# Attention chains of a fused attention and expert kernel stood in other steps, one step or more for each link

## The chip, the core and the metric

The kernel runs on one core of a Trainium2 chip. The core has five engines that run at their own pace and meet only at semaphores: PE (TensorE, matrix products, with its weight loads PEld), DVE (VectorE), ACT (ScalarE), POOL (GpSimd) and SP (SyncE, which here only starts transfers). The metric is device time of the whole program in microseconds (us); lower is better.

## What is computed

Three stages follow each other. The change concerns the first and what stands beside it.

```python
scores = scale * np.matmul(q, k.transpose(0, 1, 3, 2))    # q, k, v: 4 x 8 x 576 x 64
mask = (rel >= 0) & (rel < 64)                            # each query sees 64 keys
attn = np.exp(scores - max); attn /= attn.sum(-1) + 1e-9
x = (attn @ v) laid out as 2304 x 512
x = (((x @ w1) * (x @ w2)) @ w3) @ w_out                  # w1, w2: 512 x 1024, w3: 1024 x 1024
...
out[n] = gate[n] * relu(x[n] @ ew1[e]) @ ew2[e]           # e: the best of 8 experts of row n
```

## The kernel before

**Precision.** Each large product is done three times with reduced operands: every matrix is split into a high part (the "h" tiles, written by ACT) and a low part (the "l" tiles, the difference, written by DVE or POOL), and lines 479 to 481 multiply high by high, high by low and low by high.

**Stages.** The program has a fold stage and six chunks. The fold stage multiplies w3 by w_out once (16 half products, index i from 0 to 15 in `w_order`, evicted to Wh and Wl), and beside it splits w1 and w2 in eight pieces (`hi_w12` on ACT, then `lo_w12` on DVE or POOL). Each chunk takes 384 rows of x through eight hidden tiles (`hidden_tile`, steps 0 to 7) and six row tiles (`row_tile`, steps 8 to 13). The eight experts follow after the last chunk.

**Attention beside it.** Attention is computed in blocks, four to a stage, called 0 to 3 here. The fold stage computes the four blocks that chunk 0 needs, and each chunk but the last computes those of the next: six stages with attention in all. One block is a chain over all engines: score (PE, L571) -> masks (DVE: L998 twice, L1003, L1006; these write prob and the negative maxima nmx) -> exps (ACT, L812) -> weigh (DVE, L1024 and L1026: sums and their reciprocals) -> normal (POOL, L1430) -> turn (PE, three transposes into bank 4, L583) -> turn_out (DVE, four L1016 from bank 4 to pT) -> value (PE, L595) -> value_hi (ACT, L817) and value_lo (DVE, L1030), which write the block's columns of xT.

**What sets the order.** Seven small tables by step, `scored`, `laid`, `raised`, `weighed`, `turned`, `valued` and the constant `LAST`, say which block's link is issued in which step on each engine: scored for score, laid for masks, raised for exps, weighed for weigh, turned for turn and turn_out, valued for value with its two evictions. Block 0's score stands at the stage's start, block 3's value in the middle of step 13. In the fold stage step e is the product i = e + 2. Each engine runs its instructions strictly in the order in which they are written, so an engine that waits for one link holds back all that stands behind it. `w12_steps` says after which product each of the eight splits of w1 and w2 is issued, and `w12_pool` which of them have their low part on POOL instead of DVE.

**Waits that matter here.** There is one bank for the transposes: turn of a block waits until turn_out of the block before has read it (`pt_ok`), and for normal of its own block (`p_ok`). The score of a block waits until masks of the one before has read the score banks (`masked`). On DVE, weigh stands ahead of turn_out within a step, and in the fold stage both stand behind the low parts of w3 and w1/w2 and behind the eviction of the product (`own()`). SP issues the loads in one fixed order; a load of q and k waits for a score that frees its buffer (`s_done`), a load of v for a value (`o_done`).

Of the kernel before, what the change touches and what calls it, by code (L numbers as in the profile page):

```python
# [37 lines left out]
def build(nc, B, H, S, qk_pairs, v_pairs, w1, w2, w3T_in, w_out, w_outT, w_gates, ew1, ew2, out):  # L38
# [41 lines left out]
    with ctx:  # L80
# [186 lines left out]


        def scored(e):
            return {2: 1, 5: 2, 8: 3}.get(e)  # L270

        def laid(e):
            return {0: 0, 3: 1, 6: 2, 9: 3}.get(e)

        def raised(e):
            return {1: 0, 4: 1, 7: 2, 9: 3}.get(e)

        def weighed(e):
            return {2: 0, 5: 1, 8: 2, 10: 3}.get(e)

        def turned(e):
            return {4: 0, 7: 1, 10: 2, 11: 3}.get(e)

        def valued(e):
            return {6: 0, 9: 1, 12: 2}.get(e)

        LAST = NP - 1

# [36 lines left out]
        def fold_scored(i):  # L325
            return 0 if i == 2 else scored(i - 2)
# [2 lines left out]
        w3_steps = {1: 3, 5: 4, 7: 5, 9: 6, 11: 7}  # L329


        w12_steps = [3, 6, 8, 9, 10, 12, 13, 14]
        w12_pool = (2, 4, 5)
        pool_count = lambda n: sum(i in w12_pool for i in range(n))
        assert len(w12_steps) == 2 * KD

# [10 lines left out]
        def w_count(it, n):  # L347
            return w_order.index((it, n)) + 1
# [28 lines left out]
        @block.sync  # L377
        def _(sp):
            def load_w3(it):
                if it in w3_prev:  # L380
                    sp.wait_ge(W_done, w_count(w3_prev[it], 1))
                sp.dma_start(w3r[w3_buf[it]][:, :], w3T_in[it]).then_inc(w3_loaded(it)[0], 16)

            def load_w12(i):
                _, _, wr, src, kt = w12[i]
                if i >= KD:
                    sp.wait_ge(wo_lo, KF)
                sp.dma_start(wr[:, kt * FF:(kt + 1) * FF], src[kt * P:(kt + 1) * P, :]).then_inc(w12_in[i], 16)

            def load_woT(i):  # L390
                cols = slice(2 * i * DM, (2 * i + 2) * DM)
                sp.dma_start(woT[:, cols], w_outT[i]).then_inc(woT_in[i], 16)

            def load_wo(n, i):
                c = n * (KF // 2) + i
                sp.dma_start(wo[:, c * DM:(c + 1) * DM], w_out[c]).then_inc(wo_in[c], 16)

            load_w3(0)
            load_wo(0, 0)
            load_wo(0, 1)  # L400
            load_w3(1)
            load_wo(0, 2)
            load_wo(0, 3)
            load_w3(2)
            sp.dma_start(wgg[:, :], w_gates).then_inc(wg_in, 16)
            load_woT(0)
            load_woT(1)
            load_w3(3)
            load_woT(2)
            load_woT(3)  # L410

            def load_qk(G):
                if G >= 2:
                    sp.wait_ge(s_done, 2 * (G - 1))
                sp.dma_start(qk[G % 2][:, :], qk_pairs[G]).then_inc(qk_in[G % 2], 16)

            def load_v(G):
                if G >= 2:
                    sp.wait_ge(o_done, G - 1)
                sp.dma_start(vv[G % 2][:, :], v_pairs[G]).then_inc(v_in[G % 2], 16)  # L420

            load_qk(0)
            for i in range(KF // 2):
                load_wo(1, i)
            load_qk(1)
            load_v(0)
            load_w12(0)
            load_v(1)
            load_qk(2)
            load_w12(1)  # L430
            load_w3(4)
            load_qk(3)
            load_w3(6)
            load_w12(2)
            load_w3(5)
            load_w12(3)
            load_w12(4)
            load_qk(4)
            load_w12(5)
            load_v(2)  # L440
            load_w3(7)
            load_w12(6)
            load_qk(5)
            load_w12(7)
            load_v(3)
            load_v(4)
            load_v(5)
            for G in range(NP, len(PLACES), NP):
                for load, ahead in ((load_qk, 2), (load_qk, 3), (load_qk, 4), (load_v, 2),
                                    (load_qk, 5), (load_v, 3), (load_v, 4), (load_v, 5)):  # L450
                    if G + ahead < len(PLACES):
                        load(G + ahead)


            def load_piece(e, c):
                if c < NP1:
                    src = ew1[bass.ds(e, 1), c * P:(c + 1) * P, :].rearrange("o p f -> p (o f)")
                else:
                    j = 2 * (c - NP1)
                    src = ew2[bass.ds(e, 1), j * P:(j + 2) * P, :].rearrange("o (j p) d -> p (o j) d", p=P)  # L460
                dst = raw[c][:, :] if c < NP1 else raw[c][:, :].rearrange("p (j d) -> p j d", d=DM)
                sp.dma_start(dst, src).then_inc(raw_in[c], 16)

            sp.wait_ge(o_done, len(PLACES))
            for c in range(2 * NP1):
                load_piece(0, c)
            with sp.Fori(1, E) as e:
                for c in range(2 * NP1):
                    sp.wait_ge(ew_lo[c // NP1], e * NP1 + (c % NP1 + 1 - NP1))
                    load_piece(e, c)  # L470
            sp.wait_ge(y_last_out, 16)
# [3 lines left out]
        def _(pe):  # L475
# [149 lines left out]
            def chunk(cc, c, b, final):  # L625
# [43 lines left out]
                for f in range(KF):  # L669
                    hidden_tile(f)  # L670
                    if b is not None:
                        attend(b, f, scored(f))
                    if final and f == 1:
                        early_ranks()
                    if final and f == 4:
                        early_ids()
                for n, tt, i in row_tiles:
                    if b is not None and KF + i == NSTEP - 1:
                        row_tile(i, n, tt, lambda: value(b, LAST))
                    else:  # L680
                        row_tile(i, n, tt)
                        if b is not None:
                            attend(b, KF + i, scored(KF + i))
                    if final and i == 1:
                        x_transposes(0, bank[7])
                    if final and i == CT:
                        last_ranks()
# [115 lines left out]
        def _(act):  # L803
# [44 lines left out]
            for i, (it, n) in enumerate(w_order):  # L848
                def own():
                    first, end = PARTS[n]  # L850
                    if i == 3:
                        act.wait_ge(g1_done, 1)
                        for j in range(0, KF, 2):
                            g = act.activation(woh_pair(j, DM, WXC), bank[4][:, j * LG:(j + 2) * LG].rearrange("p (j c) -> p j c", c=LG),
                                               ACT.Copy)
                        g.then_inc(g1_hi, 1)
                    act.wait_ge(W_done, w_count(it, n))
                    act.activation(Wh[:, it * WXC + first:it * WXC + end], w_bank(i)[:, 0:end - first],
                                   ACT.Copy).then_inc(W_hi, 1)

                if i == len(w_order) - 1:
                    value_hi(0, LAST)
                own()
                if i >= 2 and valued(i - 2) is not None:
                    value_hi(0, valued(i - 2))
                if i in w3_steps:
                    hi_w3(w3_steps[i])
                if i == 2:
                    hi_wo(1)
                if raised(i - 2) is not None:  # L870
                    exps(0, raised(i - 2))
                if i in w12_steps:
                    hi_w12(w12_steps.index(i))
# [7 lines left out]
            def chunk(cc, c, b, final):  # L881
# [12 lines left out]
                def attend(e):  # L894
                    if b is not None and valued(e) is not None:
                        value_hi(b, valued(e))
                    if b is not None and raised(e) is not None:
                        exps(b, raised(e))
# [91 lines left out]
        def _(dve):  # L990
# [76 lines left out]
            for i, (it, n) in enumerate(w_order):  # L1067
# [32 lines left out]
                if laid(i - 2) is not None:  # L1100
                    masks(0, laid(i - 2))
# [8 lines left out]
            def chunk(cc, c, b, final):  # L1110
# [4 lines left out]
                def attend(e):  # L1115
                    if b is not None and turned(e) is not None:
                        turn_out(b, turned(e), 0)
                        turn_out(b, turned(e), 1)
                    if b is not None and valued(e) is not None:
                        value_lo(b, valued(e))  # L1120
                    if b is not None and laid(e) is not None:
                        masks(b, laid(e))
# [436 lines left out]
```

## Time and profile before

| | us |
|---|---|
| median of 3 runs | 725.0 (722.15 to 725.44) |
| the profiled execution | 723.5 |
| its span, first to last instruction | 721.8 |
| PE busy | 702.3 (97%) |
| DVE busy | 368.0 (51%) |
| ACT busy | 268.2 (37%) |
| POOL busy | 113.6 (16%) |
| fold stage, start of the first product to the end of the last | about 6 to 77 |
| one chunk with attention | 62.5 |

The profile is of one execution. Its time is 1.7 us over the span, which is what lies around the first and last instruction, and 1.5 us under the median. The TensorE clock was granted in full for 0.996 of the span.

### The profile page before, as it was taken

Reading aid. Unit: us, or ns where it says so; the run is one execution under the profiler, and the core shown is the slowest. Engines: PE = TensorE matmul, PEld = TensorE weight load, DVE = VectorE, ACT = ScalarE, POOL = GpSimd, SP = SyncE. Lnnn points to the kernel's source line nnn. Section 1 sums busy time; section 2 is a strip of 40 time slices with the busy share of each in tenths; the row PEclk is TensorE's granted clock in tenths of the full one; section 3 lists DMA queues with packets and bytes.
Section 4 is the critical chain, followed back from the end, with each engine's and each line's share of the span. In section 5 each row is a group of like instructions: output and inputs, shape, how many; then the busy total and the mean of one; then the engine's idle time right before and its main releaser. Section 6 shows DMA issues by size and latency. Waiting matters only on the chain.

```text
span 721.8 us, 14724 instructions
## 1 busy us (share of the span) xinstructions
PE 702.3 (97%) x5075; PEld 638.6 (88%) x5076; DVE 368.0 (51%) x690; ACT 268.2 (37%) x651; POOL 113.6 (16%) x176
## 2 busy tenths in 40 slices
PE   8998999999999999999999999999999999999997
PEld 7898999899899989989998999888888888888885
DVE  5488455345534634653464658845456554562211
ACT  4364332234233323423332253544446544552121
POOL 7123000100100010010001001222222222222211
PEclk9999999999999999999999999999999999999999
DMA  9682212311131240123015223747275753511110
GB/s 335 245 282 82 70 52 70 112 30 48 63 100 52 71 114 26 48 67 98 24 45 182 96 73 132 266 175 229 74 222 186 231 183 124 191 34 44 32 44 29
DMA packets 29485, 82.73 MB, mean 115 GB/s; under 512 B 3645, under 2 KB 3645, under 8 KB 29440
## 3 DMA queue, kind: packets, MB, share of 16 engines
q1 hardware_dynamic: 24400, 66.63, 28.3%
q0 software_dynamic: 5040, 15.47, 6.1%
q8 instruction: 32, 0.52, 0.3%
q14 instruction: 13, 0.11, 0.0%
HBM read 72.65 MB, written 10.49 MB: 115 GB/s over the span
## 4 chain that ended last, share of the span: by engine, by line
PE 91%; DVE 5%; ACT 2%; issue 1%; DMA 1%; POOLq 0%; ACTq 0%; DVEq 0%
PE bank L479 27%; PE bank L481 25%; PE bank L480 25%; PE bank L595 3%; PE bank L571 3%; PE bank L753 3%; DVE pT L1016 2%; ACT prob L812 2%; PE bank L731 1%; PE bank L583 1%; DVE sm L998 1%; PE bank L492 1%; DVE prob L1003 1%; PE bank L713 1%; DMA w3r<-in_w3T 1%
## 5 line engine op out<-in xcount | busy, mean ns | idle before, releaser
L479 PE MATMUL bank<-Wh,abh 128*128 128x272 f32 (+1 forms) x288 | 85.4, 297 | 0.0
L481 PE MATMUL bank<-Wh,abl 128*128 128x272 f32 (+1 forms) x288 | 82.0, 285 | 0.0
L480 PE MATMUL bank<-Wl,abh 128*128 128x272 f32 (+1 forms) x288 | 81.9, 284 | 0.0
L1107 DVE TENSOR_TENSOR wbuf<-raw,wbuf 128x1024 f32 (+1 forms) x64 | 75.4, 1222 | 12.5 <-ACT wbuf L878 12.4
L1306 DVE TENSOR_TENSOR hTl<-bank,hTh 128x512 fp32r<-128x512 f32 x44 | 28.4, 686 | 97.0 <-ACT hTh L926 97.0
L1128 DVE TENSOR_TENSOR ab_f<-bank,a_sb 128x384 f32<-128x384 f32 x48 | 26.8, 558 | 99.4 <-PE bank L481 98.9
L479 PE MATMUL bank<-wbuf,hTh 128*128 (+1 forms) x176 | 70.7, 402 | 0.0
L479 PE MATMUL bank<-wbuf,xsTh 128*128 (+1 forms) x176 | 70.4, 400 | 0.0
L481 PE MATMUL bank<-wbuf,hTl 128*128 (+1 forms) x176 | 68.8, 391 | 0.0
L481 PE MATMUL bank<-wbuf,xsTl 128*128 (+1 forms) x176 | 68.6, 390 | 0.0
L480 PE MATMUL bank<-wbuf,xsTh 128*128 (+1 forms) x176 | 68.6, 390 | 0.0
L480 PE MATMUL bank<-wbuf,hTh 128*128 (+1 forms) x176 | 68.4, 389 | 0.0
L479 PE MATMUL bank<-xTh,w1h 128*128 128x384 f32 x192 | 67.1, 349 | 0.0
L1430 POOL TENSOR_TENSOR prob<-prob,rec 128x384 f32<-128x384 f32 x24 | 20.8, 867 | 286.6 <-DVE rec L1026 286.6
L481 PE MATMUL bank<-xTh,w1l 128*128 128x384 f32 x192 | 64.4, 335 | 0.0
L480 PE MATMUL bank<-xTl,w1h 128*128 128x384 f32 x192 | 64.3, 335 | 0.0
L481 PE MATMUL bank<-xTh,w2l 128*128 128x384 f32 x192 | 64.2, 334 | 0.0
L479 PE MATMUL bank<-xTh,w2h 128*128 128x384 f32 x192 | 64.1, 334 | 0.0
L480 PE MATMUL bank<-xTl,w2h 128*128 128x384 f32 x192 | 64.1, 334 | 0.0
L878 ACT ACTIVATE wbuf<-raw 128x1024 f32 (+1 forms) x64 | 64.0, 1055 | 0.0
L886 ACT ACTIVATE abh<-ab_f 128x384 fp32r<-128x384 f32 x48 | 25.2, 526 | 100.0 <-DVE ab_f L1128 100.0
L479 PEld LDWEIGHTS bank<-Wh,abh 128*128 128x128 f32 x288 | 54.2, 188 | 1.9 <-issue 0.9
(217 smaller groups left out, 1469.9 us busy)
## 6 DMA issues: line engine op xcount, KB each, us to landing
raw<-in_expert_w SPq DMA_DIRECT2D x64, 512.0 KB, 4.5
qk<-in_qk SPq DMA_DIRECT2D x24, 448.0 KB, 3.6
vv<-in_v SPq DMA_DIRECT2D x24, 384.0 KB, 3.6
x_rows<-x_sb POOLq DMA_DIRECT2D x18, 256.0 KB, 3.8
w3r<-in_w3T SPq DMA_DIRECT2D x8, 512.0 KB, 3.7
wo<-in_w_out SPq DMA_DIRECT2D x8, 256.0 KB, 8.6
woT<-in_w_outT SPq DMA_DIRECT2D x4, 512.0 KB, 8.2
w2r<-in_w SPq DMA_DIRECT2D x4, 512.0 KB, 5.8
```

The costliest lines, as they stand in the source:

```text
L479: pe.matmul(dst, lh, rh, start=first, stop=False)
L480: pe.matmul(dst, lh, rl, start=False, stop=False)
L481: return pe.matmul(dst, ll, rh, start=False, stop=last)
L571: mm = pe.matmul(score_bank(h)[r * WIN:(r + 1) * WIN, i * P:(i + 1) * P], buf[rows, r * QC + i * WIN:r * QC + (i + 1) * WIN], buf[rows, kc ...
L595: mm = pe.matmul(bank[6][r * D:(r + 1) * D, (3 * h + i) * WIN:(3 * h + i + 1) * WIN], vv[G % 2][:, (i * 4 + r * 2 + h) * D:(i * 4 + r * 2 ...
L753: mm = pe.transpose(bank[3 + n][:, (f % 4) * P:(f % 4 + 1) * P], h_sb[:, f * P:(f + 1) * P], ident[:, :])
L878: act.activation(wbuf[:, bass.ds(wcol(e, part, 0, c * PC), PC)], raw[part * NP1 + c][:, :], ACT.Copy).then_inc(ew_hi[part], 1)
L886: act.activation(abh[:, f * CH:(f + 1) * CH], ab_f[f % 2][:, :], ACT.Copy).then_inc(ab_hi, 1)
L1107: dve.tensor_tensor(wbuf[:, bass.ds(wcol(e, part, 1, c * PC), PC)], raw[part * NP1 + c][:, :], f32(wbuf[:, bass.ds(wcol(e, part, 0, c * PC ...
L1128: dve.tensor_tensor(ab_f[f % 2][:, :], hidden_bank(cc, f, 1)[:, 0:CH], a_sb[f % 2][:, :], ALU.mult).then_inc(ab_ok, 1)
L1306: dve.tensor_tensor(hTl[last][:, cols], bank[3 + n][:, :], f32(hTh[last][:, cols]), ALU.subtract).then_inc(hT_lo, 1)
L1430: pool.tensor_tensor(pv, pv, rec[:, stats(p)].unsqueeze(2).broadcast_to([P, 6, WIN]), ALU.mult).then_inc(p_ok, 1)
```

## The change

The tables of steps are changed. In a chunk, by block 0, 1, 2, 3 (a dash stands for the fixed place at the start or in step 13):

| link | before | after |
|---|---|---|
| score | -, 2, 5, 8 | -, 1, 4, 7 |
| masks | 0, 3, 6, 9 | 0, 2, 5, 8 |
| exps | 1, 4, 7, 9 | 1, 3, 6, 9 |
| weigh and normal | 2, 5, 8, 10 | 2, 4, 7, 10 |
| turn and turn_out | 4, 7, 10, 11 | 3, 6, 9, 11 |
| value | 6, 9, 12, - | 5, 8, 11, - |

```diff
         def scored(e):
-            return {2: 1, 5: 2, 8: 3}.get(e)
+            return {1: 1, 4: 2, 7: 3}.get(e)
...
-        w12_steps = [3, 6, 8, 9, 10, 12, 13, 14]
-        w12_pool = (2, 4, 5)
+        w12_steps = [4, 6, 8, 10, 11, 12, 13, 14]
+        w12_pool = (0, 1, 3, 5)
...
             load_w12(1)
+            load_qk(3)
             load_w3(4)
-            load_qk(3)
             load_w3(6)
```

The first place is DVE in a chunk, from the eviction of block 1's value (L1030) to the end of step 10 or 11. prob_72 is the probability buffer of block 3, pT_73 and pT_74 are the two targets of turn_out for block 2, pT_75 and pT_76 for block 3; L1137 and L1138 evict a row tile. Before:

```order
L1030 TENSOR_TENSOR xTl<-bank,xTh 128x2x192
L998 SCALAR_TENSOR_TENSOR sm<-bank,mask 128x384 x2
L1003 TENSOR_TENSOR prob_72<-sm 128x2x3x64
L1006 TENSOR_REDUCE nmx<-prob_72 128x6
L1137 COPY x_sb_65<-bank 128x256
L1138 COPY logits<-bank 128x16
L1024 TENSOR_SCALAR sums<-sums 128x6
L1026 RECIPROCAL rec<-sums 128x6
L1016 TENSOR_TENSOR pT_73<-bank,side 64x384 x2
L1016 TENSOR_TENSOR pT_74<-bank,side 64x384 x2
L1016 TENSOR_TENSOR pT_75<-bank,side 64x384 x2
L1016 TENSOR_TENSOR pT_76<-bank,side 64x384 x2
```

After:

```order
L1030 TENSOR_TENSOR xTl<-bank,xTh 128x2x192
L998 SCALAR_TENSOR_TENSOR sm<-bank,mask 128x384 x2
L1003 TENSOR_TENSOR prob_72<-sm 128x2x3x64
L1006 TENSOR_REDUCE nmx<-prob_72 128x6
L1137 COPY x_sb_64<-bank 128x256
L1138 COPY logits<-bank 128x16
L1016 TENSOR_TENSOR pT_73<-bank,side 64x384 x2
L1016 TENSOR_TENSOR pT_74<-bank,side 64x384 x2
L1137 COPY x_sb_65<-bank 128x256
L1138 COPY logits<-bank 128x16
L1024 TENSOR_SCALAR sums<-sums 128x6
L1026 RECIPROCAL rec<-sums 128x6
```

The turn_out of block 2 now stands ahead of the weigh of block 3 and a row tile earlier.

The second place is the fold stage, DVE and POOL. On DVE from the eviction of block 1's value; w3l, w2l and w1l are low parts, Wl is the low part of a product's eviction. Before:

```order
L1030 TENSOR_TENSOR xTl<-bank,xTh 128x2x192
L998 SCALAR_TENSOR_TENSOR sm<-bank,mask 128x384 x2
L1003 TENSOR_TENSOR prob_72<-sm 128x2x3x64
L1006 TENSOR_REDUCE nmx<-prob_72 128x6
L1037 TENSOR_TENSOR w3l_105<-w3r_101,w3h_109 128x1024
L1088 TENSOR_TENSOR Wl<-bank,Wh 128x256
L1024 TENSOR_SCALAR sums<-sums 128x6
L1026 RECIPROCAL rec<-sums 128x6
L1016 TENSOR_TENSOR pT_73<-bank,side 64x384 x2
L1016 TENSOR_TENSOR pT_74<-bank,side 64x384 x2
```

After:

```order
L1030 TENSOR_TENSOR xTl<-bank,xTh 128x2x192
L998 SCALAR_TENSOR_TENSOR sm<-bank,mask 128x384 x2
L1003 TENSOR_TENSOR prob_72<-sm 128x2x3x64
L1006 TENSOR_REDUCE nmx<-prob_72 128x6
L1088 TENSOR_TENSOR Wl<-bank,Wh 128x272
L1016 TENSOR_TENSOR pT_73<-bank,side 64x384 x2
L1016 TENSOR_TENSOR pT_74<-bank,side 64x384 x2
L1037 TENSOR_TENSOR w3l_105<-w3r_101,w3h_109 128x1024
L1044 TENSOR_TENSOR w1l<-w1r,w1h 128x1024
L1088 TENSOR_TENSOR Wl<-bank,Wh 128x256
L1024 TENSOR_SCALAR sums<-sums 128x6
L1026 RECIPROCAL rec<-sums 128x6
```

On POOL in the same stage, before:

```order
L1430 TENSOR_TENSOR prob_71<-prob_71,rec 128x384
L1430 TENSOR_TENSOR prob_72<-prob_72,rec 128x384
L1440 TENSOR_TENSOR w2l<-w2r,w2h 128x1024
L1430 TENSOR_TENSOR prob_71<-prob_71,rec 128x384
L1440 TENSOR_TENSOR w1l<-w1r,w1h 128x1024
L1430 TENSOR_TENSOR prob_72<-prob_72,rec 128x384
```

After:

```order
L1430 TENSOR_TENSOR prob_71<-prob_71,rec 128x384
L1440 TENSOR_TENSOR w2l<-w2r,w2h 128x1024
L1430 TENSOR_TENSOR prob_72<-prob_72,rec 128x384
L1440 TENSOR_TENSOR w2l<-w2r,w2h 128x1024
L1430 TENSOR_TENSOR prob_71<-prob_71,rec 128x384
L1440 TENSOR_TENSOR w2l<-w2r,w2h 128x1024
L1430 TENSOR_TENSOR prob_72<-prob_72,rec 128x384
```

The turn_out of block 2 moved ahead of two low parts and of the weigh of block 3; a low part of w1 moved ahead of that weigh on DVE; and POOL has a split behind each normal, one more than before.

The third place is PE between the fold products i = 3 and i = 4 (the difference; L571 is a score of block 1, L479 begins product 4):

```order
 L492 MATMUL bank<-wgg,woT 128x16
 L509 MATMUL bank<-xTl,w3l_108 128x256
+L571 MATMUL bank<-qk_67 64x128 x12
+L479 MATMUL bank<-xTh,w3h_109 128x272
+L480 MATMUL bank<-wol,w3h_109 128x272
```

The score of block 1 moved from behind product 4 to ahead of it. The number of instructions on PE, DVE and SP is the same before and after; one low part has gone from DVE to POOL, three of the eight splits stand one product later, and of SP's loads only that of block 3's q and k has moved past one of w3.

## Rows read from the trace of the kernel before

**Rows 1.** The page, part 1: busy us, share of the span, instructions.
```profile
PE 702.3 (97%) x5075; PEld 638.6 (88%) x5076; DVE 368.0 (51%) x690; ACT 268.2 (37%) x651; POOL 113.6 (16%) x176
```
**Rows 2.** The waits of PE: waiter, releaser, us in total, times, longest.
```profile
PE bank L583 <- DVE pT L1016: 10.8, 6, 2.7
```
**Rows 3.** The chain that ended last, one chunk: start us, us, what.
```profile
184.99 0.87 PE bank L595 x24
185.89 0.50 ACT xTh L817
...
189.37 1.85 ACT prob L812 x11
...
191.64 0.43 DVE pT L1016
...
193.85 0.55 PE bank L583 x3
...
197.23 0.85 PE bank L595 x24
```
**Rows 4.** Timeline of PE, same chunk: start us, us, instruction.
```profile
191.95 0.28 PE L481 MATMUL bank<-Wh,abl 128*128 128x256 f32 x1
```
**Rows 5.** Timeline of DVE and POOL, same chunk; brackets hold idle time before and releaser.
```profile
181.57 0.42 DVE L1137 COPY x_sb<-bank 128x256 f32<-128x256 f32 x1
...
155.45 0.83 POOL L1430 TENSOR_TENSOR prob<-prob,rec 128x384 f32<-128x384 f32 x1 [14.41 <-DVE rec L1026]
...
182.59 0.83 POOL L1430 TENSOR_TENSOR prob<-prob,rec 128x384 f32<-128x384 f32 x1 [12.43 <-DVE rec L1026]
```
**Rows 6.** The chain that ended last, same chunk, hidden steps.
```profile
162.50 0.18 PE bank L481
162.67 0.33 PE bank L583 x3
```
**Rows 7.** Timeline of PE at the end of the fold stage.
```profile
64.28 0.28 PE L481 MATMUL bank<-xTl,w3l 128*128 128x272 f32 x1
67.28 0.71 PE L583 MATMUL bank<-ident,prob 128*128 128x128 f32 x3 [2.71 <-DVE pT L1016]
...
72.14 0.92 PE L595 MATMUL bank<-pT,vv 128*64 128x64 f32 x24
```
**Rows 8.** Windows: stretch, its us, PE, PEld, DVE, ACT, POOL busy (x instructions), clock, DMA.
```profile
68.00:70.00 2.00, 2.00 (x11) 2.00 (x11) 1.92 (x4) 0.00 (x0) 0.29 (x1) 0.50 0.00 0
...
194.00:196.00 2.00, 2.00 (x18) 2.00 (x18) 1.52 (x3) 0.00 (x0) 0.00 (x0) 1.00 0.34 131
```
**Rows 9.** Timeline of DVE and POOL in the fold stage.
```profile
49.06 2.28 DVE L1003 TENSOR_TENSOR prob<-sm 128x384 f32<-128x384 f32 x1
...
61.82 1.22 DVE L1037 TENSOR_TENSOR w3l<-w3r,w3h 128x1024 fp32r<-128x1024 f32 x1
64.34 0.42 DVE L1088 TENSOR_TENSOR Wl<-bank,Wh 128x256 fp32r<-128x256 f32 x1 [1.31 <-ACT Wh L858]
...
64.99 2.24 DVE L1016 TENSOR_TENSOR pT<-bank,side 64x384 f32<-64x384 f32 x4
...
48.53 2.40 POOL L1440 TENSOR_TENSOR w2l<-w2r,w2h 128x1024 fp32r<-128x1024 f32 x1 [2.08 <-ACT w2h L829]
...
65.15 0.83 POOL L1430 TENSOR_TENSOR prob<-prob,rec 128x384 f32<-128x384 f32 x1 [4.25 <-DVE rec L1026]
```
**Rows 10.** Groups by line: busy us, mean ns of one, idle before.
```profile
L1044 DVE TENSOR_TENSOR w2l<-w2r,w2h 128x1024 fp32r<-128x1024 f32 x3 | 3.7, 1223 | 2.4 <-ACT w2h L829 2.4
...
L829 ACT ACTIVATE w2h<-w2r 128x1024 fp32r<-128x1024 f32 x4 | 4.2, 1049 | 0.0
```
**Rows 11.** Timeline of DVE behind block 1's value in the fold stage.
```profile
58.80 0.56 DVE L1030 TENSOR_TENSOR xTl<-bank,xTh 128x384 fp32r<-128x384 f32 x1 [0.51 <-ACT xTh L817]
```
**Rows 12.** Timeline of PE between the fold products 3 and 5.
```profile
28.68 0.36 PE L479 MATMUL bank<-xTh,w3h 128*128 128x272 f32 x1 [1.06 <-DVE wol L1052]
...
31.85 0.89 PE L571 MATMUL bank<-qk 64*64 64x128 f32 x24
```

More of the change, by code:

```diff
@@ L269, in scored @@
         def scored(e):
-            return {2: 1, 5: 2, 8: 3}.get(e)
+            return {1: 1, 4: 2, 7: 3}.get(e)
         def laid(e):
-            return {0: 0, 3: 1, 6: 2, 9: 3}.get(e)
+            return {0: 0, 2: 1, 5: 2, 8: 3}.get(e)
         def raised(e):
-            return {1: 0, 4: 1, 7: 2, 9: 3}.get(e)
+            return {1: 0, 3: 1, 6: 2, 9: 3}.get(e)
         def weighed(e):
-            return {2: 0, 5: 1, 8: 2, 10: 3}.get(e)
+            return {2: 0, 4: 1, 7: 2, 10: 3}.get(e)
         def turned(e):
-            return {4: 0, 7: 1, 10: 2, 11: 3}.get(e)
+            return {3: 0, 6: 1, 9: 2, 11: 3}.get(e)
         def valued(e):
-            return {6: 0, 9: 1, 12: 2}.get(e)
+            return {5: 0, 8: 1, 11: 2}.get(e)
         LAST = NP - 1
```

## Prediction, written before the changed kernel was run

> **What bounds the kernel now.** The page's first part comes first: PE is busy for 97% of the span, no other engine for more than 51% [rows 1]. So a change of order can only give what PE does not do while it waits, and the clock it loses by waiting. The waits of PE come next: one group holds nearly all, L583, the transposes of a block (turn), which wait six times for DVE's L1016, turn_out of the block before; 10.8 us together, 2.7 the longest [rows 2]. Six is the number of stages with attention. The other wait that matters is a single one of 1.06 us in the fold stage [rows 12].
>
> The chain of waits says what is late in a chunk [rows 3]. Value of block 1 ends at 185.9, and from there the chain leaves PE: ACT's and DVE's evictions, masks of block 3, the six exps that end at 191.2, the weigh behind them, and only then, from 191.6, turn_out of block 2, whose transposes had long been done. Turn of block 3 starts at 193.85, when that frees bank 4. The cause is order: DVE has turn_out(2) behind weigh(3), which needs block 3's exps. The last matmul ahead starts at 191.95 [rows 4]; at its rate (about 0.12 to the next) turn would start at 192.1. The loss is 1.75 us. All five chunks with attention show this chain with the same spacing.
>
> In the fold stage the last matmul starts at 64.28 and turn at 67.28, a loss of 2.9 us [rows 7]. There it costs more: behind it the granted clock is 0.50 (1.2 GHz) from 68 to 70, while it is 1.00 (2.4 GHz) behind the chunk's 1.75 us [rows 8]. From turn to the next value lie three transposes and 24 matmuls of 256 columns in both places: 72.14 less 67.28 is 4.9 us in the fold [rows 7], 197.23 less 193.85 is 3.4 us in the chunk [rows 3]. The slow clock costs about 1.5 us.
>
> **The chunks.** PE's work is the same; two groups of small matmuls now follow each other at step 11 instead of standing apart, which costs nothing and may save one gap of 0.2 us; I take zero. Turn_out(2) now stands at step 9, behind turn(2), two row tiles (24 matmuls at 0.12 each, 2.9 us) ahead of turn(3), and takes 2.3 us [rows 9]; `pt_ok` cannot be late. What is late next is `p_ok`: exps(3), weigh(3), normal(3). Masks(3) now follows value(1) at step 8. From the value's end to the last exp the chain of before takes 191.2 - 185.9 = 5.3 us [rows 3], while weigh(3) at step 10 comes behind two row tiles, turn(2) and an eviction, 6.3 us and more behind the value. Weigh is then limited by its place, not by exps. From DVE's eviction of a row tile to the end of normal takes 182.59 + 0.83 - 181.57 = 1.85 us [rows 5]; with a hop from PE to DVE p is ready 2.0 us into step 11, and turn(3) comes after that step's row tile, 24 x 0.12 = 2.85 us. A margin of 0.8 us.
>
> The other links are nearer too. Block 0 has now one hidden tile between weigh and turn instead of two: normal(0) ends at 156.3 [rows 5], or 0.8 us later with the score that now stands ahead; turn(0) of before came at 162.67 and comes a tile (24 x 0.175 = 4.2 us) earlier, near 158.5 [rows 6]. Margin over 1 us. At step 2 DVE has both weigh(0) and masks(1), some 2.1 us more; the product ab_f of tile 3 may start some 0.1 us later on DVE, and PE needs it a whole tile later. SP's loads of q, k and v are released a step earlier, or at the same one, in the order in which they stand, and needed three or more steps (over 9 us) after that.
>
> So 5 x 1.75 = 8.75 us, and not under 8.0, (10.8 - 2.7) / 5 = 1.6 for each as the waits count them [rows 2].
>
> **The fold stage, first half.** Score(1) takes 0.8 us and stood between products 4 and 5. Now it stands before product 4, where PE waits 1.06 us for DVE's L1052 anyway [rows 12]; masks(0), for which it waits, is a product back on DVE, ahead of that L1052. Gain 0.8 us. If that cover were gone it would be zero. The load of q and k(3) waits for this score and is now ahead of w3(4), but score(1) ends before the product that w3(4) waits for, so that load is not held.
>
> **The fold stage, turn(3).** Ahead of it PE has the same work less the 0.8 us: turn(3) could start at 64.4 - 0.8 = 63.6. When is p ready? Value(1) comes one product and a score earlier, 4.0 us, so its L1030 ends at 59.36 - 4.0 = 55.4 [rows 11] and masks(3) follows: L998 until 56.3. Then L1003, which takes 0.56 us in a chunk, took 2.28 us once, ending 0.4 us after a POOL split that ran from 48.53 to 50.93 [rows 9]. The new order puts such a split there: hi_w12 of piece 3 on ACT behind value_hi(1), 1.05 us [rows 10], to 55.7, POOL's low part 2.4 us to 58.1. So L1003 ends at 58.5 and nmx at 59.05. Behind it DVE is a queue that never waits: Wl 0.35, turn_out(2) 2.25, w3 low 1.2, w1 low 1.2 [rows 10], Wl, sums and reciprocal 0.8 (64.34 to 65.15), normal 0.85 [rows 9]. 59.05 + 0.35 + 2.25 + 1.2 + 1.2 + 0.8 + 0.85 = 65.7. ACT keeps up (exps to 61.2, hi 1.05 to 62.3, before DVE wants it at 62.8).
>
> Turn(3) starts at 65.7 instead of 67.28: 1.55 us earlier, the 0.8 of score(1) included. PE still waits 2.1 us there, now for `p_ok`. **Does the clock fall?** It fell after 2.9 us and not after 1.75 in five places [rows 7, 8]; 2.1 is nearer to 1.75, so I take it that it stays, +1.5 us. It is the least sure term. The Trainium skill ("TensorE: Matmul & The Clock Gate", Part 1) says that the monitor behind the clock runs freely and is not started by the kernel, so that the moment of a change varies from run to run; by that the same wait may cost the 1.5 us in one run and not in the next. No row here shows it, as there is one execution.
>
> The skill's "SBUF" page ("Who interferes with whom") speaks against the POOL part of this change: a DVE instruction with two SBUF inputs contends with a POOL instruction that reads SBUF. The row of 2.28 us agrees. Without that blocking the queue on DVE would start 1.7 us sooner but wait for ACT's exps and split later on, p would be ready at about 65.0, and the sum would be 0.7 us better.
>
> **The sum.** 8.75 + 1.55 + 1.5 = 11.8 us. Against the profiled execution, 723.5 - 11.8 = 711.7. The median of the runs is 1.5 us above that execution, so against it 713.2. I take the middle, 712.5.
>
> **Rivals.** *The clock falls in the fold all the same.* For: the wait stays near 2 us. Gain 10.3, time 714.0. Chance 0.33; the forecast itself 0.45.
>
> *The wait only moves to p_ok in the chunks.* Turn(3) needs exps, weigh and normal of its own block; a margin of 0.8 us over a chain of four engines is thin, and DVE or POOL might be held by something that before did not show (a normal holds POOL for 0.83 us, and L1003 waits for POOL). Against: in a chunk POOL has only its normals there. If half the wait stays, 0.9 us in each of five, the gain is 11.8 - 4.5 = 7.3, time 717.0. Chance 0.13.
>
> *More is gained.* The POOL split does not meet L1003, or DVE's queue runs shorter, and turn(3) in the fold waits under 1 us: 1 us more, 711.5. Chance 0.05.
>
> *Little changes.* The order on DVE is not what holds bank 4. Against: the chain names it, and the order after shows turn_out(2) ahead of weigh(3). Only the fold's part would be left, 722. Chance 0.02.
>
> *Slower than before.* Weigh(3) on DVE holds all behind it, turn_out(3) too. If normal(3) came later than I reckon, the first 0.8 us would be free and the rest PE's wait, in each of five chunks. Breaking even needs a wait of 1.75 us and a fifth of the fold's 3.05 more, 2.35, so it decides from a normal(3) that is 3.2 us late. At 3.7 us late the wait is 2.9 us, the one at which the clock fell: 5 x (2.9 + 1.5 - 1.75) - 3.05 = 10.2 us slower, 735. The nearest price is L1003's 1.7 us of blocking [rows 9], half of that. Chance 0.02.
>
> **How the numbers follow.** 712.5 is the likeliest case. The range 709.5 to 717.5 takes in the fallen clock, the gap of 1.5 us between execution and median in both directions and the lower edge of the second rival. A change below 0.5%, 3.6 us, is about what a measurement of this kernel cannot tell from none: faster 0.95, same 0.03, slower 0.02.
>
> **What would show it.** In the profile after: the group L583 <- L1016 is gone from PE's waits in the chunks; the chunk's period falls from 62.5 to 60.7; one wait of about 2 us for POOL's normal is left in the fold at about 65.7; a score stands at 27.6 and product 4 still starts at 28.7; L1003 at about 56.3 takes 2 us; the clock is 1.00 or 0.50 in 66 to 70. Wrong would be: turn(3) of a chunk waiting for POOL, or a turn(0) that waits at step 3.

## The result and the profile after

The changed kernel takes 712.35 us (median of 4 runs, 711.21 to 713.14) against 725.17 us before (722.15 to 725.44, 4 runs): a ratio of 0.983, 95% interval 0.980 to 0.986. The profiled execution took 712.7 us, its span is 711.0 us. That is 1.7% faster; the forecast was 712.5.

The busy time of each engine in the changed kernel, on the page ([rows 1] for before):

```profile
PE 701.0 (99%) x5075; PEld 637.6 (90%) x5076; DVE 367.8 (52%) x689; ACT 267.9 (38%) x651; POOL 113.7 (16%) x177
```

DVE has one instruction fewer than before and POOL one more: the low part that changed its engine. (The text ahead of the prediction calls DVE's number the same; it is not.)

And the shares of its chain of work:

```profile
PE 97%; issue 1%; POOL 1%; DMA 1%; ACT 0%; DVE 0%; POOLq 0%; ACTq 0%; DVEq 0%
```

PE's busy time is nearly what it was (702.3 before). What is gone is idle time. The waits of PE after, all of them (before: [rows 2]; the second and third are at the program's start and were there before, the fourth is the 1.1 us of [rows 12]):

```profile
PE bank L583 <- POOL prob L1430: 2.3, 1, 2.3
PE bank L557 <- DVE prob L1060: 1.5, 1, 1.5
PE bank L525 <- DVE wol L1052: 1.0, 1, 1.0
PE bank L479 <- DVE wol L1052: 0.2, 1, 0.2
```

Six waits for DVE's turn_out have become one wait for POOL's normal, in the fold stage. The chunk that [rows 3 to 5] show reads like this after. First PE's timeline (start in us, duration in us, line; the first L583 is turn of block 2, the second of block 3, and no bracket means no wait):

```profile
182.75 0.49 PE L583 MATMUL bank<-ident,prob 128*128 128x128 f32 x3
...
188.93 0.49 PE L583 MATMUL bank<-ident,prob 128*128 128x128 f32 x3
189.35 0.92 PE L595 MATMUL bank<-pT,vv 128*64 128x64 f32 x24
```

DVE's timeline in the same chunk:

```profile
183.37 2.27 DVE L1016 TENSOR_TENSOR pT<-bank,side 64x384 f32<-64x384 f32 x4
...
186.84 0.17 DVE L1024 TENSOR_SCALAR sums<-sums 128x6 f32<-128x6 f32 x1
```

And POOL's:

```profile
187.32 0.83 POOL L1430 TENSOR_TENSOR prob<-prob,rec 128x384 f32<-128x384 f32 x1 [9.55 <-DVE rec L1026]
```

Turn_out of block 2 is done at 185.6, over three microseconds before turn of block 3. Normal of block 3 ends at 188.15, and turn starts at 188.93, 0.78 us later. The chunk's period, from one stage's first score to the next's, fell from 62.46 us to 60.52. The first scores in the chain that ended last, before:

```profile
139.78 0.82 PE bank L571 x24
202.25 0.82 PE bank L571 x24
```

and after:

```profile
136.64 0.82 PE bank L571 x24
197.16 0.81 PE bank L571 x24
```

The fold stage at the same place, on PE (before: [rows 7]):

```profile
66.16 0.52 PE L583 MATMUL bank<-ident,prob 128*128 128x128 f32 x3 [2.32 <-POOL prob L1430]
```

On DVE (before: [rows 9]):

```profile
56.56 2.28 DVE L1003 TENSOR_TENSOR prob<-sm 128x384 f32<-128x384 f32 x1
...
59.69 2.27 DVE L1016 TENSOR_TENSOR pT<-bank,side 64x384 f32<-64x384 f32 x4
61.99 1.23 DVE L1037 TENSOR_TENSOR w3l<-w3r,w3h 128x1024 fp32r<-128x1024 f32 x1
63.13 1.22 DVE L1044 TENSOR_TENSOR w1l<-w1r,w1h 128x1024 fp32r<-128x1024 f32 x1
64.38 0.42 DVE L1088 TENSOR_TENSOR Wl<-bank,Wh 128x256 fp32r<-128x256 f32 x1
64.72 0.16 DVE L1024 TENSOR_SCALAR sums<-sums 128x6 f32<-128x6 f32 x1
```

On POOL:

```profile
56.03 2.39 POOL L1440 TENSOR_TENSOR w2l<-w2r,w2h 128x1024 fp32r<-128x1024 f32 x1 [1.90 <-ACT w2h L829]
65.19 0.83 POOL L1430 TENSOR_TENSOR prob<-prob,rec 128x384 f32<-128x384 f32 x1 [6.77 <-DVE rec L1026]
```

And the stretch behind it (row of the windows; the third figure from the right, ahead of the DMA's share, is the granted clock; before: [rows 8]):

```profile
68.00:70.00 2.00, 2.00 (x11) 2.00 (x11) 1.96 (x4) 1.23 (x2) 0.33 (x1) 0.50 0.60 172
```

DVE has no bracket here: it is a queue without a gap from masks to weigh, and the block's weigh stands at its end. The clock is at 0.50 (1.2 GHz) from 68 to 70, as before.

The first hidden tile starts at 76.86 instead of 78.08 (PE's timeline, before, then after):

```profile
78.08 0.44 PE L479 MATMUL bank<-xTh,w1h 128*128 128x384 f32 x1
```

```profile
76.86 0.44 PE L479 MATMUL bank<-xTh,w1h 128*128 128x384 f32 x1
```

So of the 10.8 us by which the span fell, 1.2 come from the fold stage and 9.6 from the five chunks with attention, 1.93 each. The medians differ by 12.8 us, 2 us more; the median of before is 1.7 us above its profiled execution, that of the changed kernel 0.4 us below. The last experiment returns to that gap.

### The profile page after: what moved, and what is told of

Its sections match the earlier page's. It is cut to its first block, busy times and chain, and to the rows that moved or that the text cites. A ratio compares the mean times of both kernels' runs of the same rounds, so it can differ in the third digit from the quotient of the medians.

```text
span 711.0 us, 14724 instructions
## 1 busy us (share of the span) xinstructions
PE 701.0 (99%) x5075; PEld 637.6 (90%) x5076; DVE 367.8 (52%) x689; ACT 267.9 (38%) x651; POOL 113.7 (16%) x177
## 4 chain that ended last, share of the span: by engine, by line
PE 97%; issue 1%; POOL 1%; DMA 1%; ACT 0%; DVE 0%; POOLq 0%; ACTq 0%; DVEq 0%
PE bank L479 28%; PE bank L481 27%; PE bank L480 27%; PE bank L595 3%; PE bank L571 3%; PE bank L753 3%; PE bank L731 1%; PE bank L583 1%; PE bank L492 1%; DMA w3r<-in_w3T 1%; PE bank L713 1%; PE bank L509 0%; PE bank L507 0%; POOL w2l L1440 0%; PE bank L525 0%
## 5 line engine op out<-in xcount | busy, mean ns | idle before, releaser
L479 PE MATMUL bank<-Wh,abh 128*128 128x272 f32 (+1 forms) x288 | 84.7, 294 | 0.0
L479 PE MATMUL bank<-wbuf,hTh 128*128 (+1 forms) x176 | 70.7, 402 | 0.1
L479 PE MATMUL bank<-wbuf,xsTh 128*128 (+1 forms) x176 | 70.4, 400 | 0.1
L479 PE MATMUL bank<-xTh,w1h 128*128 128x384 f32 x192 | 67.6, 352 | 0.0
L479 PE MATMUL bank<-xTh,w2h 128*128 128x384 f32 x192 | 64.1, 334 | 0.0
L480 PE MATMUL bank<-xTl,w2h 128*128 128x384 f32 x192 | 64.1, 334 | 0.0
L1016 DVE TENSOR_TENSOR pT<-bank,side 64x384 f32<-64x384 f32 x96 | 53.2, 554 | 13.8 <-PE bank L583 12.4
```

The lines of the kernel that those rows point to most:

```text
L479: pe.matmul(dst, lh, rh, start=first, stop=False)
L480: pe.matmul(dst, lh, rl, start=False, stop=False)
L1016: cut = dve.tensor_tensor(pT[buf_of(p, h)][w * WIN:(w + 1) * WIN, :].rearrange("p (i r c) -> p i r c", r=2, c=WIN), bank[4][rows, 0:3 * P] ...
```

## The experiments

"Before" in each comparison is the kernel before, run again on the same chip beside it (medians 724.2, 724.5 and 724.9 us).

**Part of the change alone: one entry.** The kernel before with turn of block 2 a step earlier.

```diff
         def turned(e):
-            return {4: 0, 7: 1, 10: 2, 11: 3}.get(e)
+            return {4: 0, 7: 1, 9: 2, 11: 3}.get(e)
```

> The kernel before with one entry changed: turn and turn_out of block 2 at step 9 instead of 10, all other links where they were. Theory (turn_out of block 2 must stand ahead of the weigh of block 3, but masks of block 3 must also come earlier, since on DVE turn_out now stands ahead of value_lo and masks of the same step): turn_out(2) takes 2.3 us ahead of masks(3), the exps and the weigh slip by as much, and turn(3) waits for POOL's normal instead: 1.6 us of the 1.75 stay in each chunk, 0.3 us are gained in the fold stage. 724 us, the chunk's period 62.3. Rival (the order of turn_out and weigh is the whole cause, and the other links need not move): the wait is gone, 716 us, period 60.7.

Measured: 727.2 us, ratio 1.003 (1.0015 to 1.0047). Slower than before, if by little. The rival that the entry alone would do is out. PE's waits are now for normal, seven of them (row of PE's waits):

```profile
PE bank L583 <- POOL prob L1430: 12.9, 7, 2.4
```

In the chunk at 184 to 200, PE's timeline:

```profile
196.87 0.52 PE L583 MATMUL bank<-ident,prob 128*128 128x128 f32 x3 [1.85 <-POOL prob L1430]
```

and DVE's:

```profile
188.27 2.27 DVE L1016 TENSOR_TENSOR pT<-bank,side 64x384 f32<-64x384 f32 x4
190.57 0.56 DVE L1030 TENSOR_TENSOR xTl<-bank,xTh 128x384 fp32r<-128x384 f32 x1
191.05 1.01 DVE L998 SCALAR_TENSOR_TENSOR sm<-bank,mask 128x384 f32<-128x384 f32 x2
```

The turn_out that has come forward pushes value_lo and masks of block 3 back by its 2.3 us, as reckoned; turn(3) waits 1.85 us, 0.2 more than before. What I had missed is the fold stage: turn of block 2 there now waits 1.29 us for its own normal, whose weigh stands behind two low parts, turn(3) another 2.36, and the first hidden tile starts at 80.74, 2.7 us later than before. Of these 2.7, 1.5 are not the edit's: in this execution the clock was 0.50 from 29 to 31, behind PE's wait of 1.06 us for L1052, while it was 1.00 behind the same wait before, and block 1's score starts at 33.49 instead of 31.85. Two of the five chunks have a low clock too, one from 388 to 390 and one here (row of the windows); the period of this one is 64.1 us instead of 62.6:

```profile
261.00:263.00 2.00, 2.00 (x11) 2.00 (x10) 1.28 (x3) 0.00 (x0) 0.00 (x0) 0.50 0.07 23
```

Three such stretches at 1.5 us are 4.5 of the 6.5 us by which this execution's span (728.3) exceeds that of before (721.8). The edit itself costs about 2 us: 0.15 in each chunk and 1.1 in the fold stage. The profiled execution is the slowest of the seven (725.3 to 730.0).

**DVE's order alone.** The kernel before with turn_out ahead of weigh in the row steps: the call of weights goes from the end of row_tile to behind attend.

```diff
-                    weights(KF + i)
...
                     row_tile(i, n, tt)
                     attend(KF + i)
+                    weights(KF + i)
```

> The kernel before with DVE's order alone changed in the row steps of a chunk: turn_out of a block ahead of the weigh of the next in the same step; PE, ACT and POOL as before. Theory: turn_out(2) starts as soon as its transposes are done (189.2), ends at 191.4, the weigh of block 3 follows to 191.8 and normal to 192.65 on the clock of the trace before, so turn(3) waits 0.55 us instead of 1.75. Gain 5 x 1.2 = 6.0: 719 us, the period 61.3, PE's wait named POOL's normal or still DVE's turn_out at 0.5 us each. Rival (bank 4 alone held turn(3)): all 1.75 us go, 716.4 us. Rival (the order on DVE was not the cause): 725 us.

Measured: 721.5 us, ratio 0.997 (0.995 to 0.999). A gain, 0.6 us in each chunk instead of 1.2. The waits of PE:

```profile
PE bank L583 <- POOL prob L1430: 5.2, 5, 1.0
PE bank L583 <- DVE pT L1016: 2.7, 1, 2.7
```

DVE's timeline, turn_out and the weigh behind it:

```profile
188.98 2.27 DVE L1016 TENSOR_TENSOR pT<-bank,side 64x384 f32<-64x384 f32 x4
191.28 0.17 DVE L1024 TENSOR_SCALAR sums<-sums 128x6 f32<-128x6 f32 x1
```

In the chunks no wait is left on turn_out; the chain has passed to normal, and turn(3) waits 1.04 us for it. I had reckoned 0.55. On DVE the evictions of a row tile (L1137, L1138, at 188.56 and 188.90) stand ahead of turn_out(2), so that it starts, counted from the stage's first score, 0.3 us later than I had it. The rest is the way from turn_out to normal, 0.15 us longer than reckoned, and 0.15 us from the end of normal (192.59) to turn (192.74); against it stands 0.1 us by which I had turn ready too early. So the order was a cause, as the chain said, but moving it alone leaves over half of the wait: block 3's masks must come forward as well.

**The chunks without the fold stage.** The changed kernel with the fold stage of before; the argument True takes all six links' steps from the tables of before.

```diff
-                    attend(0, i - 2, fold_scored(i))
+                    attend(0, i - 2, fold_scored(i), True)
-        w12_steps = [4, 6, 8, 10, 11, 12, 13, 14]
-        w12_pool = (0, 1, 3, 5)
+        w12_steps = [3, 6, 8, 9, 10, 12, 13, 14]
+        w12_pool = (2, 4, 5)
```

> The changed kernel with the fold stage of before: its attention tables, the steps of the splits of w1 and w2, their engines and the order of the loads; the chunks as in the changed kernel. It splits the gain between chunks and fold stage. Theory as the traces of both kernels now read (the first hidden tile starts at 78.08 before and 76.86 after, so the fold stage gives 1.2 us and the chunks the rest): 713.6 us, first hidden tile at 78.1, periods 60.5. Rival (the terms of the prediction, 3.05 us in the fold stage): 715.4 us.

Measured: 713.95 us (4 runs, 712.98 to 714.07), 1.6 us over the changed kernel by the medians, with intervals of the ratios that overlap (0.984 to 0.987 against 0.980 to 0.986). The traces settle it: the first hidden tile starts at 78.24 and the period is 60.52, so 9.6 of the 10.8 us between the two spans have nothing to do with the fold stage. By the medians this kernel is 10.2 us under the runs of before beside it (724.2).

**Weigh first.** The changed kernel; in the fold stage weigh stands at the head of its step on DVE.

```diff
                 def own():
+                    if weighed(i - 2) is not None:
+                        weigh(0, weighed(i - 2))
                     if i - 1 in w3_steps:
...
-                    if weighed(i - 2) is not None:
-                        weigh(0, weighed(i - 2))
```

> The changed kernel with one move on DVE in the fold stage: the weigh of a block at the head of its product's step, ahead of the low parts of w3, w1 and w2 and of the product's eviction. Theory (turn(3) of the fold stage waits for DVE's queue, not for the exps): the exps end at 61.5 and DVE is free at 62.0, so weigh ends at 62.4 and normal at 63.3, turn(3) starts at 63.7 instead of 66.16 with no wait, and the clock stays at 1.00: 2.45 + 1.5 us gained, 708.4 us, first hidden tile at 72.9. Rival (the clock falls at that place whatever PE waits there): 709.9 us. Rival (ACT's exps or splits are the limit): 712.4 us.

Measured: 709.5 us, ratio 0.980 (0.978 to 0.981). Turn(3) starts at 64.26, the first hidden tile at 73.49, the clock stays. The wait was DVE's queue, not the exps. In none of the five executions is the mean clock under 0.999. The wait is 0.49 us and not zero (PE's timeline):

```profile
64.26 0.52 PE L583 MATMUL bank<-ident,prob 128*128 128x128 f32 x3 [0.49 <-POOL prob L1430]
```

DVE's timeline:

```profile
62.23 1.20 DVE L1037 TENSOR_TENSOR w3l<-w3r,w3h 128x1024 fp32r<-128x1024 f32 x1
```

POOL's timeline:

```profile
62.39 1.72 POOL L1430 TENSOR_TENSOR prob<-prob,rec 128x384 f32<-128x384 f32 x1 [4.05 <-DVE rec L1026]
```

Normal takes 1.72 us instead of 0.83: DVE's low part of w3, two inputs in SBUF, started 0.16 us ahead of it, and now it is POOL that is held.

**Value apart from turn.** The changed kernel with the value of block 2 at step 12.

```diff
         def valued(e):
-            return {5: 0, 8: 1, 11: 2}.get(e)
+            return {5: 0, 8: 1, 12: 2}.get(e)
```

> The changed kernel with the value of block 2 one step later (step 12, as before), so that turn(3) and value(2) stand apart again. Theory (the chunk's period fell by 1.94 us and not by the 1.75 of the wait because two groups of small matmuls now follow each other and one change between small and large products is saved): the period rises by 0.2 us to 60.7, 1.1 us in all with the fold stage, 713.5 us. Rival (the wait itself was 1.94 us long and standing together saves nothing): the period stays 60.5, 712.4 us.

Measured: 712.4 us, the same. The period is 60.61 us (75.49 to 136.10) against 60.52, so standing together gives 0.09 us, not 0.2, below what the total can show. The profile has another finding: turn(3) in the fold stage waited 2.33 us, as in the changed kernel, and this time the clock stayed at 1.00 (PE's timeline, then a row of the windows). The five executions of this one kernel are not alike: three have a mean clock of 1.000 (711.8 to 712.4 us), two 0.996 (713.0).

```profile
66.98 0.52 PE L583 MATMUL bank<-ident,prob 128*128 128x128 f32 x3 [2.33 <-POOL prob L1430]
```

```profile
68.00:70.00 2.00, 2.00 (x19) 2.00 (x19) 1.91 (x5) 0.00 (x0) 1.19 (x1) 1.00 0.03 8
```

**Piece 3 on DVE.** `w12_pool = (0, 1, 5)` in the changed kernel.

> The changed kernel with the low part of piece 3 of w1 and w2 on DVE instead of POOL. Theory (DVE's L1003 took 2.28 us at 56.6 in the fold stage because POOL's split held it up): L1003 takes 0.56 us again and nmx is ready 1.7 us earlier, DVE has 1.25 us more in its queue ahead of the weigh of block 3, so turn(3) starts 0.45 us earlier, at 65.7, with a wait of 1.85 us. If the clock stays at 1.00 after that wait (it stayed after 1.75 and fell after 2.3 and 2.7): 710.4 us; if it falls: 711.9 us. Rival (L1003 is slow for another reason): it still takes over 2 us, turn(3) starts at 67.4, 713.6 us.

Measured: 711.15 us, ratio 0.982 (0.980 to 0.983). L1003 is at its usual length and turn(3) waits 1.74 us, where I had 1.85; yet the clock fell behind this shorter wait (DVE's timeline, PE's timeline, and a row of the windows):

```profile
56.22 0.56 DVE L1003 TENSOR_TENSOR prob<-sm 128x384 f32<-128x384 f32 x1
```

```profile
65.24 0.52 PE L583 MATMUL bank<-ident,prob 128*128 128x128 f32 x3 [1.74 <-POOL prob L1430]
```

```profile
66.00:68.00 2.00, 2.00 (x26) 1.88 (x23) 1.94 (x4) 0.88 (x2) 1.41 (x1) 0.50 0.03 8
```

**How much slack a chunk has.** The changed kernel with one and with three more POOL instructions ahead of block 3's normal in each of the five chunks. The diff is that with one; with three it has range(3).

```diff
+                if b > 0 and p == NP - 1:
+                    for _ in range(1):
+                        pool.tensor_scalar(pv, pv, 1.0, None, ALU.mult).then_inc(extra_ok, 1)
+                        extra_n[0] += 1
+                        pool.wait_ge(extra_ok, extra_n[0])
```

> The changed kernel with one more POOL instruction (a product with 1.0 in place, same size as the normal) ahead of the normal of block 3 in each of the five chunks with attention. Theory (in a chunk the normal of block 3 ends 0.78 us before turn(3) can start): at 0.5 to 0.9 us for the added instruction turn(3) waits 0 to 0.15 us, 712.4 to 713.2 us. Rival (no slack): 5 x 0.5 to 0.9 us more, 715 to 717 us.

> As the run with one added POOL instruction ahead of the normal of block 3 in each chunk, with three of them. Theory (0.78 us of slack, then one for one): at 0.8 us each turn(3) waits 1.6 us in each chunk for POOL's normal, about as long as it waited for bank 4 before: 5 x 1.6 = 8 us more, 720 us, and the clock stays at 1.00 there. Rival (the normal is not on the path, or other work takes the wait up): 712.4 us. Rival (such a wait lowers the clock): 5 x (1.6 + 1.5), 728 us.

Measured: 714.7 us with one and 736.7 us with three. The added instruction takes 1.17 us, with its hop 1.25, more than I had allowed. With one turn(3) waits (4.8 - 2.3) / 5 = 0.5 us, with three 3.0 (the first number counts the fold stage's 2.3 us too; the edit moves L583 to L584). The row of PE's waits with one:

```profile
PE bank L584 <- POOL prob L1436: 4.8, 6, 2.3
```

PE's timeline with three:

```profile
131.46 0.52 PE L584 MATMUL bank<-ident,prob 128*128 128x128 f32 x3 [3.00 <-POOL prob L1436]
```

and the row of the windows behind it:

```profile
134.00:136.00 2.00, 2.00 (x11) 2.00 (x11) 0.85 (x2) 0.00 (x0) 0.00 (x0) 0.53 0.66 197
```

The waits fit 1.25 - 0.78 = 0.47 and 3 x 1.25 - 0.78 = 2.97, but the periods say more. With one the period is 61.20 us, 0.68 over 60.52, and with three 65.20, 4.68 over it, of which 1.5 are the clock: behind the wait of 3.0 us it fell in all five chunks. So the usable slack is 1.25 - 0.68 = 0.57 us, and again 3.75 - 3.18 = 0.57, not 0.78: turn cannot start before about 0.15 us after the end of normal. Beyond that the path lengthens one for one.

With three, 5 x 4.68 = 23.4 us over 712.4 are 735.8, and 736.7 was measured; in the last chunk the clock stayed low twice as long as in the others (it is still 0.50 from 396 to 398). This kernel is slower than before (ratio 1.017, 1.014 to 1.019), by 12.2 us where the prediction's last rival had 10.2 for a normal 3.7 us late: that slow side exists.

With one, 5 x 0.68 = 3.4 us show as only 2.4 in the total, because here the clock stayed at 1.00 in the fold stage, behind the same wait of 2.33 us (row of the windows):

```profile
68.00:70.00 2.00, 2.00 (x19) 2.00 (x19) 1.95 (x4) 1.04 (x2) 0.38 (x1) 1.00 0.60 190
```

Three of its four executions have a mean clock of 1.000 (714.7 us), the fourth 0.998 (716.0).

**Weigh first, and piece 3 on DVE.** Both edits together.

> The changed kernel with weigh at the head of each step of the fold stage and the low part of piece 3 on DVE instead of POOL. Theory (with weigh first turn(3) of the fold stage still waits 0.49 us for POOL's normal, because POOL's split of piece 3 holds L1003 and with it the exps): nmx is ready 1.7 us earlier, turn_out(2) ends at 61.5, weigh and normal at 62.8, turn(3) starts at 63.8 with no wait: 0.5 us less than with weigh first alone, 709.0 us, first hidden tile at 73.0. Rival (DVE's longer queue, 1.25 us more ahead of the weigh, takes the gain back): 709.5 us or more.

Measured: 709.0 us (708.58 to 709.41), ratio 0.978 (0.976 to 0.980), the lowest median of all, though its runs overlap with those of weigh first (709.02 to 710.10). Turn(3) starts at 63.60 without a wait, the first hidden tile at 72.80. What PE waits for is then only the program's start and 0.3 us for L1052.

**The changed kernel again.**

> The changed kernel once more, unaltered. Theory (the clock falls after turn(3)'s wait in the fold stage in some executions and not in others, as the run with one added normal showed: the same wait of 2.3 us, clock 1.00, first hidden tile at 75.42): the runs lie between 711 and 714 us, spread by about 1.4 us, the first hidden tile at 75.4 or 76.9. Rival (the fold stage's clock is the same in every execution): first hidden tile at 76.9 again.

Measured: 712.3 us (5 runs, 712.14 to 712.75). Turn(3) waited 2.33 us, the clock fell, the first hidden tile is at 76.33; it is earlier than 76.86 because this execution begins its first score 0.5 us earlier. The spread of 1.4 us that I expected did not show; five runs within 0.6 us do not look like two values, and their mean clocks are 0.996 to 0.998.

Other kernels do show both outcomes. Every execution has its mean granted clock on record, and a stretch at 0.50 such as that of the fold stage lowers it by 0.002. (So the 0.996 told for the kernel before is a mean, not a share of the span at full clock; a second low stretch lies at the very end, behind the last product, where it costs nothing.) The 32 executions of the kernel before that stood beside the experiments:

| mean clock | executions | us |
|---|---|---|
| 1.000 | 2 | 722.1, 722.5 |
| 0.998 | 7 | 722.0 to 724.5 |
| 0.996 or 0.997 | 14 | 723.3 to 724.9 |
| 0.993 or 0.994 | 9 | 725.0 to 726.3 |

The first row leaves no room for a low stretch, so the clock stayed even behind the fold stage's wait, which is 2.7 us in all three traces with this fold stage. The fold stage of before in the changed kernel shows the same: 1.000 in one execution of four (713.0 us against 713.9 to 714.1). The last row has at least one low stretch more than the profiled execution with 0.996; the waits in the chunks, the one at L1052 and those at the program's start are left for it. So for one and the same kernel the clock falls in some executions and not in others. That is the likely reason why the median of before in the first comparison stood above its profiled execution; the clocks of those four executions are not on record. Which wait it struck in an execution without a trace is not shown.

## Why the prediction was right, point by point

**What bounds the kernel: right.** PE's busy time moved by 1.3 us, the span by 10.8, and the waits for turn_out are gone.

**The chunks: right in mechanism, the term too small.** I had 5 x 1.75 = 8.75 us; it was 5 x 1.93 = 9.6. Of the difference of 0.18 a chunk 0.09 is the gap that I took as zero (value apart from turn), 0.03 is my rounding (191.95 + 0.12 to 193.85 is 1.78), and 0.05 may be a slower restart of PE after an idle time, 3.31 us from turn(3) to the next value before against 3.26 with value apart. The next thing to be late was `p_ok`, as named: normal ends 0.78 us ahead of turn where I had 0.8, and 0.57 of it can be used. Turn(0) with one tile between waits nowhere.

**Why one link alone does not do.** The prediction argued each link's step by itself. Two partial kernels show what single moves of turn and turn_out are worth: DVE's order alone gives 0.6 us a chunk, the turn alone takes 0.15. Both leave block 3's masks behind value(1) at step 9, and the exps, weigh and normal behind them are then the longer chain. That the links of blocks 0 to 2 other than turn_out(2) had to move too is not shown; no run moves block 3's chain by itself.

**The fold stage's start: right.** Score(1) went into PE's wait: 1.06 us became 0.24. Counted from the first score, which in this execution is 0.22 us later (20.41 instead of 20.19), product 4 starts as before (28.90 and 28.68) and product 5 comes 0.9 us sooner (32.00 and 32.67), where I had 0.8.

**Turn(3) in the fold stage: right.** Reckoned 65.7 with a wait of 2.1, measured 66.16 with 2.32; 0.22 us of the start is that of the whole execution. L1003 took 2.28 us behind POOL's split, and the queue on DVE had the members and the lengths of the sum.

**The clock: wrong.** The term was +1.5 us, on the step "2.1 is nearer to 1.75, so it stays"; measured 0. The rival with 0.33 had this right. The step failed because it took the length of the wait as what decides, and read that from one execution. Over all profiles, with the time from turn(3) to the first hidden tile beside it:

| kernel | wait at turn(3), us | clock behind it | turn(3) to hidden tile, us |
|---|---|---|---|
| before | 2.71 | fell | 10.8 |
| order of DVE alone, and fold stage of before | 2.72 | fell | 10.8 |
| one entry alone | 2.36 | fell | 10.6 |
| changed | 2.32 | fell | 10.7 |
| changed, again | 2.33 | fell | 10.7 |
| value apart | 2.33 | stayed | 9.25 |
| one more on POOL | 2.33 | stayed | 9.23 |
| three more on POOL | 2.33 | fell | 10.7 |
| piece 3 on DVE | 1.74 | fell | 10.7 |
| weigh first | 0.49 | stayed | 9.23 |
| both | 0 | stayed | 9.20 |

The price of 1.5 us was right (the last column, 10.7 less 9.2), the condition not. The two that stayed have the same fold stage up to turn(3) as the changed kernel, and the one with a POOL instruction added in the chunks has the same fold stage altogether, as has the one with three, where it fell. In the chunks 1.63 us (five times, before) left the clock alone, 1.85 us let it fall in two of five, 3.0 us in all five. I should have priced it as a chance, and then the gain in the fold stage would have been the forecast's least firm 1.5 us in the number too.

**The total.** The two errors were of opposite sign: +0.85 in the chunks, -1.85 in the fold stage. The sum against the profiled execution was 711.7 and 712.7 was measured; with the fallen clock the text had 714.0, less the 0.85 that the chunks gave more. That 712.5 met the median to 0.2 us is partly luck. I also carried the 1.5 us between execution and median over to the changed kernel; there the profiled execution is 0.4 us above the median.

## What to carry to other kernels

When an in-order engine holds a short release (here turn_out, which frees a bank) behind a step that waits for a longer chain, put the release first, but reckon the whole chain again at once: moving one link alone passed the wait to the next, and in one case made it longer. Among what is ready on a queue, put the small instruction that another engine waits for ahead of bulk work with far deadlines; moving weigh ahead of two low parts gave 2.8 us that the tables had not, about half of it in clock. A wait of PE may cost 1.5 us again in clock: here it did so behind 1.06 us in one trace of the four that have that wait and behind 3.0 us each time. Count it as a chance, remove the wait rather than shorten it, and do not read the chance from one execution.

## What the runs showed of the hardware

- The granted clock fell to 0.50 behind waits of 1.06 us (one entry alone) and 1.74 us, and stayed at 1.00 behind 2.33 us in two other kernels. In the changed kernel, value apart, one more on POOL and piece 3 on DVE, PE had been busy without a gap for several microseconds ahead of that wait, so neither the length of the last wait nor that tells which way it goes. The same kernel went both ways: the kernel before has 2 executions of 32 with a mean clock of 1.000, though its trace shows 0.50 behind 2.7 us. The text before the result named the Trainium skill's page "TensorE: Matmul & The Clock Gate", Part 1, for a monitor that runs on its own time, so that the moment of a change varies from run to run. These executions agree with it, but they do not prove it.
- DVE and POOL hold each other both ways. POOL's split held DVE's L1003 (two inputs in SBUF) for 1.7 us, and DVE's low part of w3 held POOL's normal, 1.72 us instead of 0.83. In each of these rows the one that began second was held (L1003 at 56.56 behind the split at 56.03; normal at 62.39 behind the low part at 62.23, with weigh first). L1016 and L1088, which read a bank and one SBUF tile, kept their 0.55 and about 0.4 us beside POOL.
- On POOL a tensor_scalar over 128x384 took 1.17 us and a tensor_tensor of the same size 0.83 (both in place on prob, with one more on POOL).
